# Seven products of quarters for two token tiles of x @ w_in, the last three output steps by output tiles, and w3 @ w_out in halves

## The reference

```python
# q, k, v: (2, 8, 768, 64); attention output as x: (1536 tokens, 512)
h = x @ w_in;  g = np.maximum(0.01 * h, h);  y = g @ w_out      # 512 -> 2048 -> 512
a = y @ w1;  b = y @ w2;  out = (a * b @ w3) @ moe2_w_out       # 512 -> 1024 -> 1024 -> 512
```

## Time and profile before

| | |
|---|---|
| median of 3 runs | 530.35 us (530.29 to 530.83) |
| the profiled execution: its own time, its span | 530.87 us, 529.0 us |
| TensorE busy | 523.3 us, 99% |
| VectorE, ScalarE, GpSimd busy | 259.7, 172.2, 92.6 us |
| DMA | 43.85 MB, mean 83 GB/s |

### The profile page before, as it was taken

One profiled execution on the slowest core, in us unless ns is written; L12 is line 12 of the kernel. 1 busy time (PEld: TensorE's weight loads), 2 busy tenths in 40 slices (PEclk: granted clock), 3 DMA queues, 4 the chain that ended last, 5 costly groups with the idle time before them and its releaser, 6 DMA issues.

```text
span 529.0 us, 9085 instructions
## 1 busy us (share of the span) xinstructions
PE 523.3 (99%) x3652; PEld 431.7 (82%) x3652; DVE 259.7 (49%) x387; ACT 172.2 (33%) x299; POOL 92.6 (17%) x89
## 2 busy tenths in 40 slices
PE   8999999999999999999999999999999999999997
PEld 6888888888888888888888888888888888888885
DVE  5557355655544222223324687587777653322322
ACT  5435142333433212222332335442222314232221
POOL 2213131112000000000003992222222200000000
PEclk9999999999999999999999999999999999999999
DMA  8997673441410000000001111002111111105002
GB/s 288 350 400 261 204 255 100 154 156 54 120 60 21 0 0 1 0 1 0 1 0 42 59 41 59 18 32 71 41 42 40 41 40 40 41 5 195 0 1 79
DMA packets 22344, 43.85 MB, mean 83 GB/s; under 512 B 3344, under 2 KB 3352, under 8 KB 22304
## 3 DMA queue, kind: packets, MB, share of 16 engines
q1 hardware_dynamic: 19824, 35.66, 19.9%
q10 hardware_dynamic: 2448, 7.62, 4.3%
q0 software_dynamic: 32, 0.00, 0.0%
HBM read 38.03 MB, written 5.25 MB: 82 GB/s over the span
## 4 chain that ended last, share of the span: by engine, by line
PE 98%; DMA 1%; ACT 0%; SPq 0%; DVE 0%; issue 0%
PE acc L989 14%; PE acc L990 14%; PE acc L991 14%; PE hid L989 13%; PE hid L990 12%; PE hid L991 12%; PE hid L1212 5%; PE hid L1213 5%; PE hid L1211 5%; PE hid L1022 1%; PE hid L1037 1%; PE hid L1050 1%; DMA stage<-weights 1%; PE hid L1061 1%; PE acc L1061 0%; PE acc L1050 0%
## 5 line engine op out<-in xcount | busy, mean ns | idle before, releaser
L989 PE MATMUL acc<-g_hi,wb 128*128 128x512 f32 x286 | 111.7, 391 | 0.0
L990 PE MATMUL acc<-g_lo,wb 128*128 128x512 f32 x286 | 111.3, 389 | 0.0
L991 PE MATMUL acc<-g_hi,wb 128*128 128x512 f32 x286 | 111.3, 389 | 0.0
L989 PE MATMUL hid<-xy_hi,wa_hi 128*128 128x512 f32 x256 | 100.0, 391 | 0.0
L991 PE MATMUL hid<-xy_hi,wa_lo 128*128 128x512 f32 x256 | 99.6, 389 | 0.0
L990 PE MATMUL hid<-xy_lo,wa_hi 128*128 128x512 f32 x256 | 99.6, 389 | 0.0
L840 DVE TENSOR_TENSOR g<-g,hid 128x512 f32<-128x512 f32 (+1 forms) x48 | 33.0, 687 | 102.4 <-ACT g L634 102.3
L634 ACT ACTIVATE g<-hid 128x512 f32<-128x512 f32 (+1 forms) x48 | 28.7, 598 | 128.3 <-PE hid L991 128.3
L766 DVE TENSOR_TENSOR g_lo<-g,g_hi 128x512 fp32r<-128x512 f32 (+1 forms) x64 | 50.5, 789 | 39.7 <-ACT g_hi L640 32.9
L989 PEld LDWEIGHTS acc<-g_hi,wb 128*128 128x128 f32 x286 | 53.7, 188 | 11.3
L991 PEld LDWEIGHTS acc<-g_hi,wb 128*128 128x128 f32 x286 | 53.7, 188 | 11.2
(11 more groups left out here) (129 smaller groups left out, 639.7 us busy)
## 6 DMA issues: line engine op xcount, KB each, us to landing
stage<-weights SPq DMA_DIRECT2D x88, 256.0 KB, 3.4
w_out_place<-attn ACTq DMA_DIRECT2D x12, 512.0 KB, 5.3
outT<-x_hi_place SPq DMA_DIRECT2D x11, 256.0 KB, 3.2
x_hi_place<-attn SPq DMA_DIRECT2D x4, 512.0 KB, 7.6
w_dram<-x_lo_place SPq DMA_DIRECT2D x8, 256.0 KB, 4.5
w_out_place<-attn SPq DMA_DIRECT2D x4, 512.0 KB, 8.0
stage<-w_dram SPq DMA_DIRECT2D x8, 256.0 KB, 2.7
x_lo_place<-attn SPq DMA_DIRECT2D x2, 512.0 KB, 6.8
```

Of the source, the lines that this page charges most:

```text
L989: nc.tensor.matmul(out, w_hi, a_hi, start=first, stop=False)
L990: nc.tensor.matmul(out, w_hi, a_lo, start=False, stop=False)
L991: return nc.tensor.matmul(out, w_lo, a_hi, start=False, stop=final)
```

## The change

- **Token tiles 1 and 2 of x @ w_in** come from seven products as well. Eight steps e (`first_products`, `sixth_product`, `last_product`), each making four tiles of h: two f for each of the two token tiles. The two of token tile 1 are used at once (`y_step(1, 2e-2)` and `y_step(1, 2e-1)` lie between the sixth and the seventh product and their neighbours); the two of token tile 2 get their leaky maximum at once, as one `scalar_tensor_tensor` of VectorE, and are kept unrounded (`g2`: slots of `stage`, `decay`, and slots of w_out that are read already). The third stage is then only `y_step(2, q)`, 15 in a row, with f in the order 5 to 15, 0 to 4; the rounding of g is made in it.
- **GpSimd** makes T1 to T4 of x for two halves of the columns (10 operations of 128x512 each) within the first stage, from chunk 9 on, and S1 to S4 for 16 steps in place of 8. T1 to T4 of y come after the last of the seven products of x and after y of token tile 1.
- **Weights.** The tiles of w_in are loaded a second time in pairs for the steps (`pair`, 16 tiles, the first two at f = 12 of the first stage), and five tiles of w_out again for the third stage (`out_again`). From the first pair on, `stage` has four slots in place of eight. In the third stage the roundings are placed by `OUT_AGAIN_AT`, `W34_AT`, `SPLIT_T`, `SPLIT_W12`, `SPLIT_S`.
- **w3 @ w_out** is computed in two halves of four tiles, in four banks; the first step has 4 x 3 matmuls.
- **The last three output steps** of token tile 2 (f = 5, 6, 7) are made behind the last `gate`, output tile by output tile (`add_to_out`), in place of one behind each gate.

```diff
-QUARTER = 2
-N34 = F2 * K34 // 4
+HALF = 4
+N34 = F2 * K34 // HALF
...
+STEPS = 2 * F2
...
+T_OF_X = [T2, T2, T1, T1, T3, T3, T4, T4]
...
+SPLIT_FIRST_SET = 12
+SPLIT_FIRST_SUMS = 13
+SPLIT_T_OF_X = {13: 2, 14: 4}
...
+AGAIN_OUT = 5
+LAST_ORDER = list(range(AGAIN_OUT, F1)) + list(range(AGAIN_OUT))
+OUT_AGAIN_AT = {2: 0, 3: 1, 4: 2, 5: 3, 6: 4}
+W34_AT = {4: 0, 6: 1, 7: 5, 8: 2, 9: 6, 10: 3, 11: 7, 12: 4}
+SPLIT_T = {8: [0, 1], 9: [2, 3], 13: [4, 5], 14: [6, 7]}
+SPLIT_W12 = 13
+SPLIT_S = 14
 SPLIT_AGAIN = (1, 3)
+LAST_TOGETHER = 3
...
-PRODUCTS = [(quarter, k, slot) for quarter in range(F2 // QUARTER) for k in range(K34) for slot in range(QUARTER)]
+PRODUCTS = [(part, k, slot) for part in range(F2 // HALF) for k in range(K34) for slot in range(HALF)]
...
+    return names + (set_order("pair", 0) if f == SPLIT_FIRST_SET else [])
+def last_order(q):
+    names = [("out_again", OUT_AGAIN_AT[q])] if q in OUT_AGAIN_AT else []
+    names += [("w34", W34_AT[q])] if q in W34_AT else []
+    return names + (set_order("w12", 0) if q == SPLIT_W12 else [])
...
+STAGE_LEFT = 4
+STAGED = [w % STAGE if w < PLACE["pair", 0] else (w - PLACE["pair", 0]) % STAGE_LEFT for w in range(NW)]
...
+            def first_sums(group, quarters, sums, rests):
+                (b11, b11_lo), (b12, b12_lo), _, (b22, b22_lo) = quarters
+                t1, t2 = sums[0:2]
+                made = T_STEPS * group
+                nc.gpsimd.tensor_tensor(t1, b12, b11, ALU.subtract).then_inc(t_made, 1)
+                nc.gpsimd.tensor_tensor(rests[0], b12_lo, b11_lo, ALU.subtract).then_inc(t_made, 1)
+                pool.wait_ge(t_made, made + 2)
+                nc.gpsimd.tensor_tensor(t1, t1, rests[0], ALU.add).then_inc(t_made, 1)
+                pool.wait_ge(t_made, made + 3)
+                nc.gpsimd.tensor_tensor(t2, b22, t1, ALU.subtract).then_inc(t_made, 1)
+                pool.wait_ge(t_made, made + 4)
+                nc.gpsimd.tensor_tensor(t2, t2, b22_lo, ALU.add).then_inc(t_made, 1)
...
+            pool.wait_ge(k_pow_copied, 1)
+            for c in range(NCHUNK - 1):
+                decay_keys(c)
+                decay_queries(c)
+            last = NCHUNK - 1
+            decay_keys(last)
+            pool.wait_ge(hid_ready, FIRST_SET)
+            pool.wait_ge(x_split, CREDIT_X + last - 1)
+            first_sums(*of_x(0))
+            decay_queries(last)
+            other_sums(*of_x(0))
+            weight_sums(0)
+            pool.wait_ge(x_split, CREDIT_X + NCHUNK)
+            first_sums(*of_x(1))
+            other_sums(*of_x(1))
+            for e in range(1, F2):
+                weight_sums(e)
+            pool.wait_ge(z_ready, STEPS)
...
+                first_sums(*of_y(row))
+                other_sums(*of_y(row))
+            for e in range(F2, STEPS):
+                weight_sums(e)
...
+            def leaky_of(out, exact, done):
+                nc.vector.scalar_tensor_tensor(out, exact, LEAK, exact, ALU.mult, ALU.max).then_inc(done, 1)
+            def leaky_later(f, exact):
+                if f == STAGE - STAGE_LEFT:
+                    dve.wait_ge(masked, NCHUNK)
+                elif f > AGAIN_OUT:
+                    dve.wait_ge(acc_done, CREDIT_G + F1 + g2_slot(f) + 1)
+                leaky_of(g2(f), exact, g2_ready)
+            s1, u2, u3 = joins(2)
+            for e in range(F2):
+                if e > 0:
+                    dve.wait_ge(g2_ready, 2 * e)
+                join_u2(e, s1, u2)
+                if e == 0:
+                    for j in range(j, len(T_OF_X)):
+                        t_lo(j)
+                if e + 1 < F2:
+                    for _ in range(2):
+                        weight_lo(w)
+                        w += 1
+                dve.wait_ge(scaled, F1 + e + 1)
+                nc.vector.tensor_tensor(g[:, 0, :], g[:, 0, :], bank(X_BANKS[e % 3]), ALU.max).then_inc(g_ready, 1)
+                join_u3(e, s1, u3)
+                dve.wait_ge(z_used, 2 * e + 1)
+                leaky_later(2 * e + 1, u3)
+                if e + 1 < F2:
+                    s_lo(e + 1)
+                join_s1(e, s1)
+                dve.wait_ge(g_split, F1 + 2 * e + 2)
+                leaky_of(g[:, 1, :], s1, g_ready)
+                split_hidden(F1 + 2 * e)
+                if e == 0:
+                    y_lo(0)
+                join_z(e, u2)
+                leaky_later(2 * e, u2)
+                split_hidden(F1 + 2 * e + 1)
...
+            for q, f in enumerate(LAST_ORDER):
+                split_gated(2 * F1 + q, g2(f))
+                if q == 0:
                     y_lo(1)
-                for _ in last_pass_order(f):
+                for _ in last_order(q):
                     weight_lo(w)
                     w += 1
-                if f == SPLIT_S:
-                    s_lo(0)
-                for j in SPLIT_T.get(f, []):
-                    t_lo(j)
+                if q == SPLIT_S:
+                    s_lo(F2)
+                for j in SPLIT_T.get(q, []):
+                    t_lo(len(T_OF_X) + j)
+            s1, u2, u3 = joins(1)
...
+            def first_products(e, t, x_used):
+                x_bank, y_bank, z_bank = bank(X_BANKS[e % 3]), bank(Y_BANK), bank(Z_BANKS[e % 3])
+                name = ("pair", 2 * e + 1) if e < F2 else ("w12", 2 * (e - F2) + 1)
+                pe.wait_ge(split_done, CREDIT_SPLIT + PLACE[name] + 1)
+                if e > 1:
+                    pe.wait_ge(z_used, 2 * (e - 1))
+                small_product(x_bank, e, A11, B11, t, True).then_inc(x_ready, 1)
+                pe.wait_ge(s_split, 2 * e + 1)
+                if e % F2 == 0:
+                    pe.wait_ge(t_split, 2 if e < F2 else 2 * 4 + 6)
+                if e > 0:
+                    pe.wait_ge(y_used, 3 * e)
+                small_product(y_bank, e, S2, T2, t, True).then_inc(y_ready, 1)
+                pe.wait_ge(*x_used)
+                if e == 0:
+                    pe.wait_ge(t_split, 4)
+                small_product(z_bank, e, S1, T1, t, True).then_inc(z_ready, 1)
+                pe.wait_ge(s1_copied, e + 1)
+                small_product(x_bank, e, A12, B21, t, False).then_inc(x_ready, 1)
+                pe.wait_ge(s_split, 2 * e + 2)
+                if e % F2 == 0:
+                    pe.wait_ge(t_split, 6 if e < F2 else 2 * 4 + 7)
+                pe.wait_ge(y_used, 3 * e + 1)
+                small_product(y_bank, e, S3, T3, t, False).then_inc(y_ready, 1)
+            def sixth_product(e, t):
+                if e % F2 == 0:
+                    pe.wait_ge(t_split, 8 if e < F2 else 2 * 4 + 8)
+                pe.wait_ge(y_used, 3 * e + 2)
+                small_product(bank(Y_BANK), e, A22, T4, t, False).then_inc(y_ready, 1)
+            def last_product(e, t):
+                pe.wait_ge(z_used, 2 * e + 1)
+                small_product(bank(Z_BANKS[e % 3]), e, S4, B22, t, False).then_inc(z_ready, 1)
+            pe.wait_ge(x_split, CREDIT_X + NCHUNK)
+            for e in range(F2):
+                first_products(e, 1, (g_ready, CREDIT_G + F1 + max(2 * e - 1, 0)))
+                if e == 0:
+                    y_step(0, F1 - 1)
+                else:
+                    y_step(1, 2 * e - 2)
+                sixth_product(e, 1)
+                if e > 0:
+                    y_step(1, 2 * e - 1)
+                last_product(e, 1)
+            for f in range(F1 - 2, F1):
+                y_step(1, f)
+            for q in range(F1 - 1):
+                y_step(2, q)
...
+            for f in range(F2):
+                if f + 1 < F2:
+                    if f > 0:
+                        pe.wait_ge(gate_ready, f)
+                    gate(f + 1, 0)
+                    gate(f + 1, 1).then_inc(hid_ready, 1)
+                if f < F2 - LAST_TOGETHER:
+                    out_step(NT - 1, f)
+            def add_to_out(d, f):
+                hi, lo = gated_parts(f)
+                cols = slice(d * P, (d + 1) * P)
+                pe.wait_ge(g_hi_done, N1 + 2 * F2 + f + 1)
+                nc.tensor.matmul(acc[:, d, :], wb[:, w34_slot(f), 0, cols], hi, start=False, stop=False)
+                nc.tensor.matmul(acc[:, d, :], wb[:, w34_slot(f), 1, cols], hi, start=False, stop=False)
+                pe.wait_ge(g_split, CREDIT_G + N1 + 2 * F2 + f + 1)
+                return nc.tensor.matmul(acc[:, d, :], wb[:, w34_slot(f), 0, cols], lo, start=False, stop=f + 1 == F2)
             for d in range(2):
...
+                add_to_out(d, F2 - 1).then_inc(bank_done, 1)
+            add_to_out(2, F2 - 2)
+            add_to_out(2, F2 - 1).then_inc(bank_done, 1)
+            for f in range(F2 - LAST_TOGETHER, F2):
+                last = add_to_out(KD_TILES - 1, f)
+            last.then_inc(acc_done, 1)
...
```

More of the change, by code:

```diff
@@ L144, in weight_order @@
         names += pass_order(f)
-    for f in range(F1):
-        names += last_pass_order(f)
+    for e in range(1, F2):
+        names += set_order("pair", e)
+    for q in range(F1):
+        names += last_order(q)
```

(40 more changed lines are left out.)

561 lines of the change are left out of this document (292 added, 269 removed).

## The result

The changed kernel takes 538.66 us (median of 4 runs, 537.61 to 539.69), the kernel before 530.59 us beside it (530.29 to 530.84): ratio 1.0157, 95% interval 1.0144 to 1.0169, so 1.6% slower. The forecast was 535.5 us. The profiled execution took 539.69 us, span 537.8 us: 8.8 us more span than before.

What follows compares the result with a forecast made beforehand. TensorE was taken as the bound: matmuls by their pitch, plus its waits. Saving 11.8 us and losing 16.9 made it 5.1 us slower: 530.87 becomes 536.0, or 535.5 us allowing for the profiled run's 0.5 excess; range 527 to 540.

Steps and rivals of the forecast that it cites:

- 48 matmuls: Token tiles 1 and 2 of hidden: 336 matmuls in place of 384, at 0.2267 us each; 10.9 us saved.
- w3 @ w_out in halves: Start of the kernel: the 0.63 us wait for a rounded tile at 7.85 us goes; 0.6 us gained.
- y_step(0, 8): First stage: its g_lo is delayed by up to three waits for GpSimd's sums; 1.0 us lost, bounds 0 to 2.4.
- hidden(14): First stage: VectorE's two-input operations, with pair tiles added, delay the leaky maximum it needs; 2.2 us lost, bounds 0 to 3.
- steps of x: Late VectorE roundings and a late join at steps 0 and 1, other steps hidden; 1.2 us lost, bounds 0 to 4.
- third stage to q = 9: 20 VectorE operations alternate with GpSimd's 20 sums at 1.70 us a pair, delaying g_lo; 11.5 us lost.
- short sums at q = 12 to 14: Third stage's end: GpSimd's eight short S sums meet VectorE's operations; 1.0 us lost, bounds 0 to 3.
- last three steps: Kernel's end: earlier output tiles are ready sooner, so the last DMA may meet less; 0.3 us gained.
- The sign that the prediction gave: Profile after: TensorE idle 10 to 13 us in all before third-stage y_step, q = 3 to 9, released by VectorE's g_lo.
- the third rival: Steps of x are bound by VectorE, with scalar_tensor_tensor at over 1.8 us; 544 us, chance 0.08.
- The second rival: VectorE gets more than every second turn against GpSimd, so only total work counts; 528 us, chance 0.13.
- The first: Rival: VectorE and GpSimd hinder each other by at most 1 us, so the saving stands; 519 us, chance 0.10.

Runs made afterwards that it cites:

- e1: Changed kernel with 12 of GpSimd's 20 third-stage sums of y narrowed to 16 of 512 columns, left incomplete; 526.59 us, ratio 0.9932.
- e2: Changed kernel with the 20 sums of y in the third stage made by VectorE instead of GpSimd; 530.60 us, ratio 0.9997.
- e4: Changed kernel with unread filler matmuls put where TensorE waits longest, the awaited data as late as before; 536.36 us, ratio 1.0116.
- e10: Kernel before, with five second-stage subtractions put off by 5 to 9 repeats of themselves on VectorE; 551.49 us, ratio 1.0387.
- e8: Kernel before, with w3 @ w_out in halves as the only change; 530.52 us, ratio 1.0000.
- e9: As e5, but in step 0 ScalarE scales the bank before it rounds the gate's weight sums; 523.67 us, ratio 0.9875.
- e5: As e3, with sums earlier in VectorE's order and GpSimd's second short-sum sets waiting for VectorE's last T rounding; 525.25 us, ratio 0.9908.
- e3: As e2, with the 20 sums of x in the first stage moved from GpSimd to VectorE too; 530.15 us, ratio 0.9988.
- e6: Changed kernel with only the 20 sums of x moved to VectorE, the sums of y staying on GpSimd; 537.14 us, ratio 1.0144.

## Why the prediction was right, and where it was off

That the change makes the kernel slower, and where, was right, at 1.6% in place of 1.0%; the time lies 3.2 us above the forecast, inside its bounds by 1.3. Against the profiled execution, whose span grew by 8.8 us where 5.1 were forecast, term by term (us; minus is gained):

| term | forecast | measured | from |
|---|---|---|---|
| 48 matmuls | -10.9 | -10.9 | records |
| w3 @ w_out in halves | -0.6 | +0.7 | first y step at 70.28, before 69.57 |
| `y_step(0, 8)` | 1.0 | 1.8 | 1.53 + 0.16 + 0.08 |
| `hidden(14)` | 2.2 | 2.4 | 2.20 + 0.16 + 0.08 |
| clock behind it | none | 1.6 | pitch 0.43 |
| steps of x | 1.2 | 0.6 | 0.33 + 0.16 + 0.08 |
| third stage to q = 9 | 11.5 | 11.1 | below |
| clock behind q = 9 | none | 1.6 | pitch 0.43 |
| short sums at q = 12 to 14 | 1.0 | 0 | no wait |
| last three steps | -0.3 | -0.5 | end of the span |

The measured terms add up to 8.4; 0.4 us are not assigned. Beside the clock, misses of both signs nearly cancel (0.5 us in all), which is luck.

- *The third stage*, the term that decides, is right to 0.4 us, and for the reason given. q = 1 began at 301.76 - 0.43 - 2 x 2.72 = 295.9, q = 9 at 328.83: 32.9 us for 21.8 of matmuls. GpSimd's 20 sums took from 294.82 to 328.14, 33.3 us for the 34.0 forecast. e1 shows the cause by narrowing 12 of the sums, e2 by taking them off GpSimd. Where both had work, each let the other pass after every operation, 1.70 us a pair at 512 columns and 1.15 with 256 on GpSimd. By the Trainium skill ("SBUF — State Buffer", Who interferes with whom) the pair of ports that VectorE and GpSimd share is an exclusive lock; these turns agree with it. The sign that the prediction gave, 10 to 13 us of idle time there, was set too high: the brackets add up to 8.0 us, and the 11.1 us are these, 0.24 for each of six waits, and the drop at 318.69.
- *The step that failed* is "time is the number of matmuls by their pitch, plus whatever TensorE is made to wait": a matmul behind a long wait has another pitch. Two clock drops on the path took 3.2 us of TensorE's time, against 3.7 us between forecast and result; e4 and e10 show them by themselves. But e4 also shows that they covered two waits of 0.65 us which the prediction had, so their net worth is about 1.9 us. The third drop cost nothing of its own, since TensorE would have waited there anyway.
- *The first stage.* `hidden(14)` is right. `y_step(0, 8)` was given 1.0 with a bound of 2.4 and cost 1.8; a wait costs 0.24 us more than its idle time, which no term had.
- *The steps of x, and the short sums.* `scalar_tensor_tensor` took 0.692 us, as taken, and the third rival is out. Of the two waits forecast at the start, the one at step 1 stands (0.33 us idle for 0.4), the one at step 0 and the one of the short sums only in e4, with the clock full: 0.41 us idle for 0.8 and 0.42 for 1.0. The terms were sound, and the clock drops ahead of them hid them.
- *The halves*: the wait at 7.85 us is gone, but it is not a fixed cost of the kernel before. e10 starts as that kernel does, without halves, and its trace has no such wait and reaches the first y step at 68.95. The term was read from one execution. The changed kernel's profiled execution had two waits on the way that none of the other nine profiles with halves shows at that size (0.48 and 1.03 us), which makes the +0.7; in those the first y step starts 0.3 to 1.7 us before 69.57, a spread that e10 without halves lies in. e8 puts the worth at nothing that the time can tell, within 0.5 us. No run shows the 0.6 us.
- *The second rival* (more than every second turn) is out: VectorE had exactly every second turn while both had work. *The first* (the saving stands) is out for this order of work, but e9 comes to within 5 us of it, 523.67 against 519, by giving the sums to the engine that they hinder.

## What to carry to other kernels

Handing sums to an idle GpSimd did not help VectorE here, where GpSimd's sums and VectorE's subtractions both read two operands from SBUF: count such operations on both engines as one queue. 20 of each took 33.3 us in turns; VectorE alone would make all 40 in 24.4, an estimate at 0.61 us each, and e5 and e9 show a gain. When work is taken from TensorE, look for the stage whose cover it was: here 48 matmuls fewer left a stage with 2.72 us a step for 2.5 roundings. And price a wait of TensorE with what follows it.

## What was not expected of the hardware

TensorE's clock fell to its lower level behind short waits, in the middle of 500 us of unbroken work. Over the profiles of the changed kernel and its variants and of e10, every wait of 2.18 us or more was followed by 6 to 13 matmuls at 0.43 us, 1.4 to 2.9 us lost (12 waits), and none of 1.63 us or less was. Of the 9 waits in between, 4 were, and no row tells which will be: 1.96 us at the first step of x dropped the clock in e3 and not in e6, which has the same first stage; 2.07 and 2.08 us in the changed kernel's third stage went once without and once with, and 2.15 us in e9 without.

Windows behind that wait of 1.96 us, in e3 and then in e6:

```profile
171.00:173.00 2.00, 2.00 (x7) 1.52 (x6) 2.00 (x4) 1.88 (x4) 0.00 (x0) 0.50 0.00 0
```

```profile
171.00:173.00 2.00, 2.00 (x11) 1.64 (x10) 1.93 (x4) 1.82 (x4) 0.00 (x0) 1.00 0.00 0
```

So such a kernel has several times: e2's runs at a mean granted clock of 0.996 or 0.997 took 528.1 to 529.7 us, those at 0.993 or 0.994 took 530.4 to 531.2.
